# A token mixer and routed experts on one core: fewer clearings before the first tile, unread matmuls in short waits, and two counts of the second routing search moved

## What is computed

```python
# mixer, per batch and head, for t in range(768), head_dim 40, 4 x 8 heads
m_new = max(f[t] + m, i[t]);  f_s = exp(f[t] + m - m_new);  i_s = exp(i[t] - m_new)
C = f_s * C + i_s * outer(v[t], k[t]);  n = f_s * n + i_s * k[t]
y[t] = sigmoid(o[t]) * (C @ q[t]) / max(|n @ q[t]|, 1)
# routing: x is y as 3072 rows of 320; 8 experts, 384 tokens each
logits = x @ w_gate                       # all 3072 * 8 pairs taken in falling order,
                                          # a token to the expert if both are still free
out[mask] = relu(x[mask] @ w1[e]) @ w2[e] # 320 -> 1024 -> 320, per expert
# second layer on every row: 320 -> 2048 -> 320
h = x @ w_in;  out = where(h > 0, h, exp(min(h, 0)) - 1) @ w_out
```

## Time and profile before

| | |
|---|---|
| median of 3 runs | 818.94 us (816.48 to 819.0) |
| the profiled execution | 818.66 us, its span 816.9 us |
| mean granted PE clock | 0.991 |
| PE busy | 783.7 us (96%) |
| DVE busy | 516.5 us (63%) |
| ACT busy | 470.1 us (58%) |
| POOL busy | 395.0 us (48%) |
| HBM traffic | 51.67 MB read, 8.26 MB written |

### The profile page before, as it was taken

One profiled execution on the slowest core, in us unless ns is written; L12 is line 12 of the kernel. 1 busy time (PEld: TensorE's weight loads), 2 busy tenths in 40 slices (PEclk: granted clock), 3 DMA queues, 4 the chain that ended last, 5 costly groups with the idle time before them and its releaser, 6 DMA issues.

```text
span 816.9 us, 17697 instructions
## 1 busy us (share of the span) xinstructions
PE 783.7 (96%) x6031; PEld 728.4 (89%) x6031; DVE 516.5 (63%) x1435; ACT 470.1 (58%) x1003; POOL 395.0 (48%) x470
## 2 busy tenths in 40 slices
PE   7999999989889999999999999999999999999994
PEld 6989898977788989999999989999998999999894
DVE  6667776767768657764865776577658656442441
ACT  5555555512428653883677288548827762993673
POOL 5545455535615650664266256507633651664233
PEclk9999999999999999999999999999999999999998
DMA  8989999423410211212021211112120212121000
GB/s 129 153 144 169 166 163 177 82 83 111 120 60 24 80 49 54 66 54 77 26 71 50 69 48 56 57 46 71 51 84 26 63 48 70 55 65 40 2 1 24
DMA packets 137716, 60.96 MB, mean 75 GB/s; under 512 B 104425, under 2 KB 135913, under 8 KB 137641
## 3 DMA queue, kind: packets, MB, share of 16 engines
q1 hardware_dynamic: 135224, 52.11, 29.6%
q0 software_dynamic: 2400, 7.88, 3.1%
q10 hardware_dynamic: 16, 0.01, 0.0%
HBM read 51.67 MB, written 8.26 MB: 73 GB/s over the span
## 4 chain that ended last, share of the span: by engine, by line
PE 63%; DVE 6%; ACT 5%; issue 2%; POOL 2%; SPq 0%; DMA 0%; ACTq 0%; POOLq 0%
PE bank L1940 7%; PE bank L2037 7%; PE bank L1941 6%; PE bank L1947 6%; PE bank L2039 6%; PE bank L2038 6%; PE bank L1949 3%; PE bank L1948 3%; PE bank L1993 3%; PE bank L1995 3%; PE bank L1994 3%; PE bank L1873 2%; PE bank L1981 1%; DVE unit L1612 1%; PE bank L1978 1%
## 5 line engine op out<-in xcount | busy, mean ns | idle before, releaser
L1346 POOL TENSOR_TENSOR gl_lo<-unit,gl_hi 128x384 fp32r<-128x384 f32 x128 | 130.4, 1019 | 270.0 <-ACT gl_hi L1809 269.8
L2037 PE MATMUL bank<-Wo_hi,gl_hi 128*128 128x320 f32 x384 | 125.0, 325 | 0.5 <-POOL gl_lo L1346 0.5
L2039 PE MATMUL bank<-Wo_hi,gl_lo 128*128 128x320 f32 x384 | 118.7, 309 | 0.0
L2038 PE MATMUL bank<-Wo_lo,gl_hi 128*128 128x320 f32 x384 | 118.4, 308 | 0.0
L1773 ACT ACTIVATE hid_hi<-bank 128x384 fp32r<-128x384 f32 x64 | 31.4, 491 | 129.5 <-PE bank L1949 129.5
L1609 DVE SCALAR_TENSOR_TENSOR unit<-bank,unit 128x384 f32<-128x384 f32 x104 | 57.9, 556 | 75.9 <-ACT bank L1802 75.9
L1790 ACT ACTIVATE unit<-bank 128x384 f32<-128x384 f32 x128 | 62.4, 487 | 52.8 <-PE bank L1949 43.8
L1940 PE MATMUL bank<-x_hi,Wi_hi 128*128 128x384 f32 x224 | 80.6, 360 | 2.4 <-DVE unit L1612 1.6
L1941 PE MATMUL bank<-x_hi,Wi_lo 128*128 128x384 f32 x224 | 76.2, 340 | 0.0
L2037 PEld LDWEIGHTS bank<-Wo_hi,gl_hi 128*128 128x128 f32 x384 | 72.7, 189 | 3.1 <-POOL gl_lo L1346 3.1
L1612 DVE TENSOR_TENSOR unit<-unit,bank 128x384 f32<-128x384 f32 x128 | 70.9, 554 | 4.4
(11 more groups left out here) (302 smaller groups left out, 2089.7 us busy)
## 6 DMA issues: line engine op xcount, KB each, us to landing
stage<-in_moe_w_dram SPq DMA_DIRECT2D x32, 320.0 KB, 3.0
stage<-in_moe_w_dram SPq DMA_DIRECT2D x32, 256.0 KB, 2.6
stage<-in_moe_w_dram SPq DMA_DIRECT2D x96, 64.0 KB, 2.5
k_in<-in_k_dram SPq DMA_DIRECT2D x24, 160.0 KB, 3.9
q_in<-in_q_dram SPq DMA_DIRECT2D x24, 160.0 KB, 4.4
o_in<-in_o_gate_dram SPq DMA_DIRECT2D x24, 160.0 KB, 4.0
v_in<-in_v_dram SPq DMA_DIRECT2D x24, 160.0 KB, 3.5
x_rows<-xt SPq DMA_DIRECT2D x24, 160.0 KB, 3.2
```

The source lines that it names most:

```text
L1346: nc.gpsimd.tensor_tensor(gl_lo[:, b, :], ex[:, b, :], gl_hi[:, b, :].bitcast(F32), ALU.subtract).then_inc(gl_ok, 1)
L2037: nc.tensor.matmul(acc[j][:, 0:DM], gl_hi[:, f % RG, t_], Wo_hi[:, f, :], start=(f == 0), stop=False)
L2038: nc.tensor.matmul(acc[j][:, 0:DM], gl_hi[:, f % RG, t_], Wo_lo[:, f, :], start=False, stop=False)
L2039: ins = nc.tensor.matmul(acc[j][:, 0:DM], gl_lo[:, f % RG, t_], Wo_hi[:, f, :], start=False, stop=(f == NF2 - 1))
```

## The change

- DVE's two clearings and the semaphore `cols_ok` are gone; PE and POOL wait for `cols_step` alone.
- `gather_in(0, 0)`, the transposes of tile 0, moves in front of `columns_of_rows(0)` on PE. The columns go to banks 5 and 7, since the transposes hold bank 0 and 1. `warm(7)` becomes `warm(8)`.
- The second pair of `first_columns` moves from SP's queue to POOL's, with a semaphore of its own, ahead of the load of `wg`.
- On ACT the tanh of tile 0's gates moves in front of `by_token(0)`; `high_parts(1)` moves from behind tile 0's exps into tile 1, behind its copies, and tile 1's tanh behind it.
- At the mixer's end 8 unread matmuls (`warm(2)`, `warm(1)`, `warm(2)`, `warm(3)`) stand around the last gates; in `one_round` one stands before the fold and two before the thresholds (14 in five rounds).
- `count_takers(1, 1)` moves from in front of `up(0, 2)` into its middle. Beside expert 0's second layers `count_takers(2, 1)` and `list_tokens(1)` move behind `down2` of block 7, the thresholds into block 8, and DVE's `choose_tokens` and `round_test` behind its `elu` of block 7.

```diff
-        pcols = [[bank[0][:, 0:HALF_COLS], bank[2][:, 0:HALF_COLS]], [bank[7][:, 0:HALF_COLS], bank[7][:, HALF_COLS:2 * HALF_COLS]]]
-        plast = [bank[3][:, 0:HALF_COLS], bank[7][:, 2 * HALF_COLS:3 * HALF_COLS]]
+        pcols = [[bank[n][:, 0:HALF_COLS], bank[n][:, HALF_COLS:2 * HALF_COLS]] for n in (5, 7)]
+        plast = [bank[n][:, 2 * HALF_COLS:3 * HALF_COLS] for n in (5, 7)]
...
+        def first_columns(eng, j, done):
+            for par in range(2):
+                row = par * DP + j * NP
+                eng.dma_start(exp_l[0][row:row + NP, :].bitcast(F32),
+                              parts[par:H:2, 2 + j, 0:SPAN].bitcast(F32)).then_inc(done, 16)
...
             sp.wait_ge(parts_hi, 2)
-            first_columns(0)
-            sp.wait_ge(rows_step, C_LO)
-            first_columns(1)
+            first_columns(sp, 0, exp_in[0])
             load_out_gates(0, 1, 1)
...
+            pool.wait_ge(exp_const, 2)
+            pool.wait_ge(rows_step, C_LO)
+            first_columns(pool, 1, columns_in)
             pool.wait_ge(wg_zero, 1)
             for n, (a, w) in enumerate(XK):
                 nc.gpsimd.dma_start(wg[0:w, n, 0:E], w_gate[a:a + w, :]).then_inc(wg_in, 16)
 
-            pool.wait_ge(cols_ok, 1)
             pool.wait_ge(cols_step, 3)
...
             dve.wait_ge(cols_step, 3)
-            nc.vector.memset(eA[:, :, :].rearrange("p (b c) h -> p b c h", b=B)[:, :, 0, :], 0.0)
-            nc.vector.memset(carry[:, :, :].rearrange("p (b c) n -> p b c n", b=B)[:, :, 0, :], 0.0).then_inc(cols_ok, 1)
-            dve.wait_ge(cols_ok, 1)
             tiles(dve, body)
...
             first_rows(act, 1)
+            out_gate(0, 0, 0)
             by_token(0)
...
-                act.wait_ge(out_gates_in[u], (i + 1) * 16)
-                if not (peeled(g) and g < RING):
-                    act.wait_ge(y_ok, g - RING + 1)
-                nc.scalar.activation(o_th[u][:], o_in[u][:], ACT.Tanh, scale=0.5).then_inc(th_ok, 1)
+                if not (peeled(g) and g < 2):
+                    out_gate(g, u, i)
...
+                if peeled(g) and g == 1:
+                    high_parts(1)
+                    out_gate(g, u, i)
                 for par in range(2):
                     act.wait_ge(e_pe, g * 2 + par + 1)
                     nc.scalar.activation(W[u][:, par], pE[par], ACT.Exp).then_inc(w_ok, 1)
-                if peeled(b) and b == 0 and c == 0:
-                    high_parts(1)
...
+            pe.wait_ge(const_ok, 1)
+            warm(21)
+            pe.wait_ge(pads_ok, 1)
+            gather_in(0, 0)
+            columns_of_rows(0)
+            warm(8)
+            pe.wait_ge(cols_step, 3)
+            pe.wait_ge(exp_const, 2)
+            pe.wait_ge(pads_ok, 2 * RING + 1)
...
-                    pe.wait_ge(exp_in[half], (b + 1) * EXPONENTS if half else (b + 2) * EXPONENTS)
+                    pe.wait_ge(exp_in[half], b * EXPONENTS + (EXPONENTS if half else FIRST_EXPONENTS))
+                if peeled(g) and g < 1:
+                    pe.wait_ge(columns_in, 32)
...
             rows_to_columns(G - 2, (G - 2) % RING)
+            warm(2, to=2)
             gate(G - 2, (G - 2) % RING, G - 1)
+            warm(1, to=2)
             rows_to_columns(G - 1, (G - 1) % RING)
+            warm(2, to=2)
             gate(G - 1, (G - 1) % RING, G - 1)
+            warm(3, to=2)
...
             if q in FOLDED:
                 count_parts(k, q)
+                spin(1, pX)
                 fold_parts(k, q)
             else:
                 count_takers(k, q)
+            spin(2, pX)
             count_thresholds(k, q)
...
-        count_takers(1, 1)
...
-                up(k, u)
+                up_high(k, u)
+                if first_expert(k) and u == 2:
+                    count_takers(1, 1)
+                up_low(k, u)
...
-                if after == 2 and first_expert(k) and f == count_beside(k):
-                    count_takers(c + 1, 1)
-                    list_tokens(c)
-                elif after == 2 and not first_expert(k) and f == count_beside(k) + 1:
+                if after == 2 and f == count_beside(k) + 1:
                     count_thresholds(c + 1, 1)
...
                 if after == 2 and f == count_beside(k):
-                    (count_thresholds if first_expert(k) else count_takers)(c + 1, 1)
+                    count_takers(c + 1, 1)
+                    if first_expert(k):
+                        list_tokens(c)
```

43 lines of the change are left out of this document (17 added, 26 removed).

## The result

The changed kernel took 812.18 us in the median of four runs (811.52 to 814.67), beside 818.97 (816.48 to 819.51) for the kernel before: a ratio of 0.9929, with a 95% interval of 0.9900 to 0.9958. It was run again with the experiments, and took 813.24 (812.10 to 816.05, six runs; ratio 0.9941, 0.9923 to 0.9959). The median of the ten runs is 812.8. So it is faster, by 6.8 us in the first series and by 5.6 in the second, 0.7 to 0.8%. The forecast was 811.4, with a range of 809.8 to 814.6.

A forecast was written before the change was run, and what follows sets the result against it. PE, busy in 96% of the span, was taken as the bound. Gains of 5.0 (prologue), 0.2 (count) and 2.3 (block 7) summed to 7.5 us, from 818.66 to 811.16, or 811.4 for the median; range 809.8 to 814.6.

The forecast's parts named there:

- The prologue: Before tile 2: tile 0 begins at 12.7, its scores run at full clock, and tile 2 begins 5.0 us sooner.
- The cover of the reload: Tile 3: reload of the second half's operands, last issued between 23.4 and 24.2, just fits; cost 0, at most 2.8 us.
- one of the signs that the prediction had named as wrong: Tile 0 or 3: PE waiting for exp_l or exp_r would show the prediction wrong; no size given.
- The end of the mixer: Before the last gates: two unread products fill 0.52 of a 0.57 us wait; cost 0, at most 2.1 us.
- The second search's 14 products: Search beside expert 0: unread products cost 0, fold to thresholds stays 0.69 us; upper bound 3.0 us.
- The count in `up(0, 2)`: Middle of `up(0, 2)`: four matmuls fill a 0.71 us wait; gain 0 to 0.7, taken as 0.2 us.
- Block 7: Expert 0's second layers: `down2` fills the 1.03 us wait and half clock goes; 2.3 us sooner, 0.9 if clock falls.
- The prologue gives less: Rival: half clock in tiles 0 and 1 (1.55), or tile 3 waits (up to 2.8); about 812.9 us, chance 0.17.
- More is gained: Rival: bounds of the count and transposes, and no wait of the thresholds, give up to 1.3 more; 810.1 us, chance 0.11.
- The clock did not fall in block 7: Answers the rival that block 7's clock still falls, its count and list being small matmuls; 812.8 us, chance 0.15.
- POOL's transfer was not late: Answers the rival that POOL's queue delivers late, tile 0 starting 3.6 us later than forecast; 815.0 us, chance 0.04.
- the unread products were not wholly on the path: Answers the rival that unread products at mixer's end and second search cost 5.1 us in full; 816.5 us, chance 0.05.

The follow-up runs named there:

- the run with a filled wait: The kernel before, with 15 unread products in place of 7 ahead of the first tile's transposes; 818.93 us, ratio 0.9991.
- The run with one product: Changed kernel with table store before weights, reload before tile 3's inputs, and one unread product for three behind the mixer's last gate product; 814.18 us, ratio 0.9950.

## Why the prediction held, and where its terms were off

*The prologue, forecast 5.0 us at tile 2: measured 4.61.* The steps came nearly as told: tile 0 at 12.70 (12.7), scores at 13.04 (13.2) with the clock at full, tile 2 at 20.73 (20.3). That tile 0 came to the hundredth is luck: the transposes began 0.28 late (8.99 for 8.71), took 0.13 less (up to 9.96) and the unread products 0.11 less than told, and in the nine profiled runs with this prologue tile 0 begins anywhere from 12.02 to 12.83. The clock's share was put at 1.55, and the run with a filled wait has it at 1.43. The 0.4 that is missing is in tiles 0 and 1: tile 1's transposes start at 14.81 (14.65), and from there to tile 2 it is 5.92 us, where the prediction took the columns of the second half as equal to a carried part and said 5.65. That equality was not the fault: the columns took 0.76 (17.11 to 17.87), a carried part 0.87 (22.07 to 22.94). The interval it carried over has no wait, and tile 1 waits 0.33 for POOL's product ahead of the addend; its products are also 0.17 longer. The run with the filled wait has 5.92 too (17.99 to 23.91), with a wait of 0.33 at the same place, there for ACT's copy.

*The cover of the reload, forecast 0 with a bound of 2.8: measured 0.83 in the first profiled run.* This is the step that failed, inside a forecast that held: PE waits for exp_r at tile 3, one of the signs that the prediction had named as wrong. It took the store as ready when its data are, 18.0 to 18.7, and carried it to a reload between 23.4 and 24.2. The store's place is behind the weights' four issues, and the reload's behind the inputs of tile 3, in a queue with no free time; the last reload was issued at 25.05. The landing was taken from the nearest row, 2.1 us; 2.57 passed in this run and 1.99 to 2.22 in the others, so that size was about right, and what was wrong is the issue, 0.85 to 1.65 us later than told. In the four other profiled runs with this queue order tile 3 followed tile 2 by 6.14 to 6.60 us (second run of the changed kernel 6.37), so the usual cost is 0.1 to 0.5 and 0.83 is its high end.

*The end of the mixer, forecast 0 with a bound of 2.1: measured 0.25.* The first five products fit, as the earlier trace rows said of them. Of the last three the prediction looked at PE's own wait and not at who waits behind PE: the search of DVE opens with PE's sequencer, and two of the three lie ahead of that. The run with one product gives the 0.25 back.

*The second search's 14 products, forecast 0: measured 0.* From fold to thresholds 0.71, 0.98, 0.68 and 0.98 us, as before to 0.01. With three times as many the excess is on the path, so the price that was set against it was real, only not reached.

*The count in `up(0, 2)`, forecast 0.2: 0.2 at first, 0.1 later.* From 4.22 us sooner at the start of `up(0, 0)` (206.70 for 210.92) it goes to 4.44 at the first round's thresholds and to 4.35 at the fourth's. No run has this move alone, so the 0.1 is read from the whole change.

*Block 7, forecast 2.3: measured 2.66*, from 4.31 at the last product of its `up2`, the last place ahead of what was moved, to 6.97 at the `down2`; block 7's part alone gives the same. None of the ten profiled runs with this part has the half clock in the block; three of the four without have it. The run with the filled wait, which is the fourth, splits the sum: 1.21 by the clock up to that `down2`, put at 1.42, and 1.45 by the order, put at 0.9. The order had a deduction of 0.15 for thresholds that might wait, and they do not: PE's row at 261.73 has no wait. The stop also cost more than its 1.03: from the last product of `up2` to the next instruction it is 1.37 us before and 0.17 after.

*What was not in the sum.* The kernel before had a third half-clock stretch, from 200.5 to 204.5, at expert 0's list. The profiled run of the changed kernel had not, and from the first search's products to the start of `up(0, 0)` it gained 0.70 us (3.52 to 4.22): 0.36 by a shorter wait for DVE ahead of the list, which varies from run to run, and 0.34 behind it. The profiled run of the second series had the stretch, one of nine among the fourteen. No edit of the change stands there, and the gain is of one execution; without it the first profiled run would have been at 812.2. So it is in part luck that this run came within 0.4 us of the sum. The ten runs' median, 812.8, is 1.4 above the 811.4 that was forecast for it. The terms above account for 0.4 in the prologue, 0.1 to 0.8 at tile 3, 0.25 at the mixer's end and 0.1 at the count, less 0.4 in block 7, together 0.5 to 1.2; the rest, 0.2 to 0.9, no run shows by itself. A stretch at half clock, which one run has and the next has not, is enough to cover it.

*The rivals.* "The prologue gives less" was the case that came nearest, by its late reload, with 0.1 to 0.8 us where its middle was 1.4. "More is gained" was put at 1.3, and its three bounds add up to 1.1. The clock did not fall in block 7, POOL's transfer was not late (tile 0 did not wait), the unread products were not wholly on the path, and in eight of the ten profiled runs with the change of the prologue nothing was at half in tiles 0 and 1.

## What to carry to other kernels

A store and its reload in a queue are not due when their data are ready, but when the queue comes to them: before a gain of 5 us is let through, lay that queue's issues end to end from its first busy row, since moving one forward makes another late. An unread product was free up to the length of the wait and paid past it, and the wait to compare it with is that of the last engine released behind PE, not PE's own. Two executions of one kernel can differ by 1.5 us or more through a stretch at half clock that only one has, so terms are best read place by place and the sum checked against several runs.

## What the runs showed of the hardware that was not expected

DVE and POOL held each other up in the prologue. In the kernel before POOL did not touch tile 0's k until 14.31, because it waited for the clearing of carry at DVE's end, so DVE's row work, which ended there, never met it:

```profile
14.31 0.72 POOL L393 TENSOR_TENSOR kw<-k_in,eZ 128x320 f32<-128x320 f32 x1 [4.22 <-DVE carry L575]
```

Now POOL multiplies from 12.2 to 12.5 on. In the second profiled run of the changed kernel, DVE's rows and then POOL's:

```profile
11.71 1.36 DVE L457 TENSOR_TENSOR_SCAN A_rows<-keep,a_rows 32x384 f32<-32x384 f32 x1
13.10 2.77 DVE L459 TENSOR_TENSOR c_rows<-i_rows,A_rows 32x384 f32<-32x384 f32 x1
```

```profile
12.22 1.36 POOL L394 TENSOR_TENSOR kw<-k_in,eZ 128x320 f32<-128x320 f32 x1
13.55 1.21 POOL L400 TENSOR_SCALAR_AFFINE_SELECT W<-W 128x512 f32<-128x512 f32 x2
14.74 0.71 POOL L394 TENSOR_TENSOR kw<-k_in,eZ 128x320 f32<-128x320 f32 x1
```

The subtraction at L459 takes 0.55 us alone and 2.77 here: it starts while POOL's multiply runs and ends at 15.87, 0.42 behind the last of POOL's rows at 15.45, so that hardly any of its own 0.55 lies ahead of POOL's end. POOL's multiply takes 0.72 alone and 1.36 beside the scan. The same 2.77 stood in four of the nine profiled runs with the prologue as changed; in the other five it took 0.9. What goes with it is how early tile 0 came: its exponents began at 12.02 to 12.26 in the four and at 12.44 to 12.83 in the five. In the four POOL's masks follow its multiply back to back (1.21 or 1.22 us for the two); in the five there is a pause ahead of them or between them. The Trainium skill (SBUF — State Buffer, Who interferes with whom) says that a DVE instruction with two SBUF inputs contends with a GpSimd instruction that reads SBUF, and calls the lock on the shared ports an exclusive one. The trace agrees, with 2.77 for 0.55; that DVE did not get in between POOL's instructions either, the section does not say. The prediction had used that section for the preparing of POOL's DMAs alone, and called DVE's rows there exempt; that held for the DMAs and said nothing of POOL's own arithmetic.

On PE the 2.77 cost what the earlier start had gained: in that run tile 0 began at 12.02, 0.68 before the first run's, the columns of the second half then waited 0.20 us and the next product 0.37, and tile 2 began at 20.74, as in the first run (20.73). So the earlier tile 0 gave nothing at tile 2 there. And DVE's tables, and with them the store where it stands first, come later: 19.79 and 19.91 in the two profiled runs that had the store first in the queue and met it, where 17.83 and 18.13 stood in those that did not. In these two the clock also fell, at 18.5 and 18.0, right behind waits of 0.36 us for DVE's product, and tile 2 began at 22.45 and 23.44; the second run of the changed kernel and the one without unread products had such a wait of 0.37 and kept their clock. Whether the 2.77 is what makes some executions of the changed kernel longer was not tried by itself.
